# Eight convolution steps written out, with a third slot for the routed rows

## What is computed

```
w = softmax(weight, -1)                      # 8 heads x 7 taps
x = einsum('hk,bskhg->bshg', w, windows(x))  # causal, per head
for layer in (moe, moe2):
    logits = x @ w_gate
    e = argmax(logits); gate = softmax(logits)[e]
    x = gate * (relu(x @ w1[e]) @ w2[e])     # layer 2: also * sigmoid(x @ w_output_gate)[e]
```

## Time and profile before

| | |
|---|---|
| median of 3 timed runs | 1504.32 us (1502.03 to 1505.77) |
| profiled execution | 1496.17 us, span 1494.7 us, mean granted clock 0.916 |
| PE busy | 1249.3 us (84%) |
| DVE, ACT, POOL busy | 877.8, 635.4, 461.5 us |
| HBM over the span | 114 GB/s |

### The profile page before, as it was taken

How to read it: one execution, slowest core, us unless ns; L and a number is a source line. 1 busy time by engine, 2 the same in 40 slices (tenths; PEclk the granted TensorE clock), 3 DMA queues, 4 the chain that set the end, 5 groups by cost and what they waited for, 6 DMA issues and landing times.

```text
span 1494.7 us, 38165 instructions
## 1 busy us (share of the span) xinstructions
PE 1249.3 (84%) x13162; PEld 1155.2 (77%) x13162; DVE 877.8 (59%) x2364; ACT 635.4 (43%) x1126; POOL 461.5 (31%) x485
## 2 busy tenths in 40 slices
PE   0565664249999989999999999399999999999998
PEld 0554653249888878889888888299999999999997
DVE  4577777617888878887666666533333333333333
ACT  0456655314554544555444444133333333333333
POOL 3056756721333213332222222122222222222222
PEclk9867666579999999999999999599999999999999
DMA  4455765573757464746241411425244143313520
GB/s 135 133 178 186 231 203 185 179 211 84 188 146 218 119 188 134 225 123 191 42 133 43 141 38 33 158 52 140 49 141 142 46 143 84 106 48 99 176 62 21
DMA packets 202062, 192.55 MB, mean 129 GB/s; under 512 B 146142, under 2 KB 178554, under 8 KB 195872
## 3 DMA queue, kind: packets, MB, share of 16 engines
q1 hardware_dynamic: 176352, 127.72, 31.2%
q0 software_dynamic: 24512, 62.66, 13.2%
q10 hardware_dynamic: 1152, 1.59, 0.3%
HBM read 100.93 MB, written 68.96 MB: 114 GB/s over the span
## 4 chain that ended last, share of the span: by engine, by line
PE 56%; DVE 13%; issue 12%; ACT 5%; DMA 5%; POOL 4%; another core or an unknown queue 3%; SPq 1%; DVEq 0%; POOLq 0%; ACTq 0%
PE bank L665 55%; POOL rows L471 3%; DMA stage<-in_moe_w 2%; DVE am L889 2%; DVE hl L1072 2%; ACT rT L524 1%; ACT hh L605 1%; DVE xs L893 1%; DMA xT<-rows 1%; DMA rows<-rowa,idxa 1%; PE bank L670 1%; DVE band L877 1%; DVE split L973 1%; ACT conv L524 1%
## 5 line engine op out<-in xcount | busy, mean ns | idle before, releaser
L665 PE MATMUL bank<-xT,wslot 128*128 128x256 f16 x5040 | 607.0, 275 | 59.9 <-DMA xT<-rows 53.9
L1072 DVE SCALAR_TENSOR_TENSOR hl<-bank,hh 128x512 f16<-128x512 f32 x504 | 344.1, 690 | 410.8 <-ACT hh L605 383.5
L665 PEld LDWEIGHTS bank<-xT,wslot 128*128 128x128 f16 x5040 | 488.7, 98 | 118.9 <-DMA xT<-rows 54.3
L665 PE MATMUL bank<-wslot,hh 128*128 128x192 f16 x4032 | 525.8, 247 | 10.4 <-DVE hl L1072 4.5
L665 PE MATMUL bank<-wslot,hl 128*128 128x192 f16 x2016 | 497.6, 247 | 0.0
L605 ACT ACTIVATE hh<-bank 128x512 f16<-128x512 f32 x504 | 298.2, 598 | 388.4 <-PE bank L665 381.5
L665 PEld LDWEIGHTS bank<-wslot,hh 128*128 128x128 f16 x4032 | 363.0, 98 | 21.6 <-DVE hl L1072 8.4
L512 POOL DMA_INDIRECT out_tokens<-y,idxt x126 | 122.5, 972 | 415.8 <-ACT y L616 393.8
L485 POOL DMA_INDIRECT rows<-rowt,idxp x126 | 139.3, 1105 | 278.3 <-DVE idxp L950 247.6
L665 PEld LDWEIGHTS bank<-wslot,hl 128*128 128x128 f16 x2016 | 197.8, 98 | 0.1
L616 ACT ACTIVATE y<-bank,tf 128x192 f32<-128x192 f32 x252 | 92.1, 416 | 246.9 <-PE bank L665 210.0
(11 more groups left out here) (135 smaller groups left out, 843.4 us busy)
## 6 DMA issues: line engine op xcount, KB each, us to landing
wslot<-image SPq DMA_DIRECT2D x32, 1024.0 KB, 5.4
wslot<-image SPq DMA_DIRECT2D x32, 768.0 KB, 7.4
image<-split SPq DMA_DIRECT2D x8, 1024.0 KB
image<-split POOLq DMA_DIRECT2D x8, 1024.0 KB
xw<-in_x SPq DMA_DIRECT2D x4, 1536.0 KB, 13.2
stage<-in_moe_w SPq DMA_DIRECT2D x8, 768.0 KB
image<-split SPq DMA_DIRECT2D x8, 768.0 KB
stage<-in_moe_w POOLq DMA_DIRECT2D x8, 768.0 KB, 9.0
```

The lines of the kernel that those rows point to most:

```text
L665: return nc.tensor.matmul(o, a, b_, start=start, stop=stop, skip_group_check=True)
L1072: V.scalar_tensor_tensor(hl[:, c, :], bank[c][:, :], 0.0, hh[:, c, :], ALU.max, ALU.subtract).then_inc(hl_out, 1)
```

## The change

`steps` is a plain Python loop, so that all eight steps are straight code on every engine; the arithmetic that tied DVE's link semaphore to a loop counter goes. `rowa` and `idxa` get SLOTS = 3 slots, used as n % 3, with two scatter semaphores each; ACT's wait before its copies of step n is for the scatter of n-3 where it was n-2. For space, `xs` lies in slot 0 of `wslot` and the third `rowa` slot in slot 1 of it; the expert phase gets a small buffer `xsl` for its own scaled rows; and SP waits for the last step's `lo_ready` before the first load into `wslot`.

```diff
+SLOTS = 3
-        xs = sb("xs", [P, G, D], f32)
-        rowa = sb("rowa", [P, 2, G, RW], f32)
+        xsl = sb("xsl", [P, W2T, D], f32)
+        rowab = sb("rowab", [P, 2, G, RW], f32)
-        idxa = sb("idxa", [P, 2, G], i32)
+        idxa = sb("idxa", [P, SLOTS, G], i32)
         wslot = sb("wslot", [P, 2, WCOL], f16)
+        xs = wslot[:, 0, :].bitcast(f32)[:, 0:G * D].rearrange("p (w d) -> p w d", d=D)
+        rowa = [rowab[:, 0, :, :], rowab[:, 1, :, :],
+                wslot[:, 1, :].bitcast(f32)[:, 0:G * RW].rearrange("p (w c) -> p w c", c=RW)]
-        scat_a = [sem(f"scat_a{i}") for i in range(4)]
+        scat_a = [sem(f"scat_a{i}") for i in range(2 * SLOTS)]
         def steps(eng, body):
-            for q in range(SPB):
-                body(q, 0, q)
-            with eng.Fori(1, B) as b:
-                for q in range(SPB):
-                    body(b * SPB + q, b, q)
+            for n in range(STEPS):
+                body(n, n // SPB, n % SPB)
...
                     sp.wait_ge(dump_stored, 32)
+                    sp.wait_ge(lo_ready, STEPS)
...
                 for w in range(G):
                     nc.gpsimd.indirect_dma_start(
-                        rows[0][:, :], bass.IndirectOffsetOnAxis(idxa[0:WIN, q, w:w + 1], 0),
-                        rowa[0:WIN, q, w, :], None, bounds_check=ROWS - 1, oob_is_err=False).then_inc(scat_a[2 * q + w // (G // 2)], 16)
+                        rows[0][:, :], bass.IndirectOffsetOnAxis(idxa[0:WIN, n % SLOTS, w:w + 1], 0),
+                        rowa[n % SLOTS][0:WIN, w, :], None, bounds_check=ROWS - 1,
+                        oob_is_err=False).then_inc(scat_a[2 * (n % SLOTS) + w // (G // 2)], 16)
...
-            for i in range(4):
-                pool.wait_ge(scat_a[i], 8 * G * B)
+            for i in range(2 * SLOTS):
+                pool.wait_ge(scat_a[i], 8 * G * len(range(i // 2, STEPS, SLOTS)))
...
                 for half in range(2):
-                    if late(n, 2):
-                        act.wait_ge(scat_a[2 * q + half], b * 8 * G)
+                    if late(n, SLOTS):
+                        act.wait_ge(scat_a[2 * (n % SLOTS) + half], n // SLOTS * 8 * G)
                     ws = slice(half * G // 2, (half + 1) * G // 2)
-                    last = copy(rowa[0:WIN, q, ws, :].bitcast(f16)[:, :, 0:D], xs[0:WIN, ws, :])
+                    last = copy(rowa[n % SLOTS][0:WIN, ws, :].bitcast(f16)[:, :, 0:D], xs[0:WIN, ws, :])
...
-            dve_steps(n_here[0])
+            steps(dve, step)
```

More of the change, by code:

```diff
@@ L60 @@
 PER_QUAD = ((38, 40), (0, 0))
-PER_BATCH = 34
 EXPMASK = 0x7F800000
@@ L458, in step @@
                 if late(n, 1):
-                    scatter_step(n - 1, 1 - q)
+                    scatter_step(n - 1)
                 weight_maxima(n, q)
@@ L465, in weight_maxima, with scatter_step @@
                 nc.gpsimd.partition_all_reduce(wmx[:, slot, :], wam[:, slot, :], P, RMAX).then_inc(wmax_all, 1)
-            def scatter_step(n, q):
+            def scatter_step(n):
                 pool.wait_ge(index_ready, n + 1)
@@ L623, in row_hi @@
                         act.wait_ge(scat_p[v], i * 16 * W2T)
-                    copy(rowt[:, v, 0:n, :].bitcast(f16)[:, :, 0:D], xs[:, 0:n, :]).then_inc(hi_ready, 1)
+                    copy(rowt[:, v, 0:n, :].bitcast(f16)[:, :, 0:D], xsl[:, 0:n, :]).then_inc(hi_ready, 1)
                 def row_T(p, r):
@@ L706, in step, with step_logits @@
                 if late(n, 1):
-                    step_logits(n - 1, 1 - q)
-            def step_logits(n, q):
+                    step_logits(n - 1)
+            def step_logits(n):
                 def round_logits(r):
@@ L724, in step_logits @@
                     for i in range(RT):
-                        last = transposes(lambda c: dst[:, c, i, :], rowa[0:WIN, q, r * RT + i, :].bitcast(f16))
+                        last = transposes(lambda c: dst[:, c, i, :], rowa[n % SLOTS][0:WIN, r * RT + i, :].bitcast(f16))
                     last.then_inc(rT_done, 1)
@@ L738, in _ @@
             step_ranks(STEPS - 2)
-            step_logits(STEPS - 1, 1)
+            step_logits(STEPS - 1)
             step_ranks(STEPS - 1)
@@ L892, in scale_rows, with low_rows @@
             def scale_rows(nrows, nwins, src):
-                return V.scalar_tensor_tensor(xs[0:nrows, 0:nwins, :], src, CX,
+                return V.scalar_tensor_tensor(xsl[0:nrows, 0:nwins, :], src, CX,
                                               inv[0:nrows, 0:nwins].unsqueeze(2).broadcast_to((nrows, nwins, D)), ALU.mult, ALU.mult)
-            def low_rows(nrows, nwins, row):
-                V.tensor_tensor(row[:, :, D:D + DB], xs[0:nrows, 0:nwins, P:D], row[:, :, P:D], ALU.subtract)
-                return V.tensor_tensor(row[:, :, D + DB:2 * D], xs[0:nrows, 0:nwins, 0:P], row[:, :, 0:P], ALU.subtract)
+            def low_rows(scaled, row):
+                V.tensor_tensor(row[:, :, D:D + DB], scaled[:, :, P:D], row[:, :, P:D], ALU.subtract)
+                return V.tensor_tensor(row[:, :, D + DB:2 * D], scaled[:, :, 0:P], row[:, :, 0:P], ALU.subtract)
             def choose(nrows, nwins, bank_logits, gated):
@@ L985, in step_place @@
             def step_place(n, q):
-                factor(WIN, G, q, False, n + 2, rowa[0:WIN, q, :, MF:MF + 1])
+                factor(WIN, G, q, False, n + 2, rowa[n % SLOTS][0:WIN, :, MF:MF + 1])
                 dve.wait_ge(rank_done, n + 1)
-                place(WIN, G, rank_bank(G, RA), None, idxa[0:WIN, q, :]).then_inc(index_ready, 1)
+                place(WIN, G, rank_bank(G, RA), None, idxa[0:WIN, n % SLOTS, :]).then_inc(index_ready, 1)
             def step(n, b, q):
@@ L1007, in step @@
                 dve.wait_ge(hi_ready, n + 1)
-                row32 = rowa[0:WIN, q, :, :]
+                row32 = rowa[n % SLOTS][0:WIN, :, :]
                 V.tensor_copy(row32[:, :, MI:MI + 1], ids[0:WIN, :].unsqueeze(2))
-                low_rows(WIN, G, row32.bitcast(f16)).then_inc(lo_ready, 1)
+                low_rows(xs[0:WIN, :, :], row32.bitcast(f16)).then_inc(lo_ready, 1)
                 weights_max(q, None, None, 1)
@@ L1103, in low_out @@
                     V.tensor_copy(rowt[:, v, 0:n, MI:MI + 1], tidp[:, 0:n].unsqueeze(2))
-                    low_rows(P, n, rowt[:, v, 0:n, :].bitcast(f16)).then_inc(lo_ready, 1)
+                    low_rows(xsl[:, 0:n, :], rowt[:, v, 0:n, :].bitcast(f16)).then_inc(lo_ready, 1)
                 def choose_out(p):
```

2 lines of the change are left out of this document (1 added, 1 removed).

## The result

The changed kernel took 1495.26 us, the median of four runs (1491.05 to 1497.29), the kernel before 1505.05 (1502.03 to 1507.06) beside it: a ratio of 0.9933, 95% interval 0.9905 to 0.9961. That is 9.8 us less, where 1492.8 was predicted.

A forecast was written before the change was run, and what follows sets the result against it. Waits bound the convolution phase, TensorE the expert phase. Gains of 2.19 (step 2) and 9.34 (steps 3 to 5), together 11.5 us, took 1496.17 to 1484.7 profiled and the median 1504.32 to 1492.8 us; range 1481 to 1503.

The forecast's parts named there:

- (a): Steps 2, 4, 6, 7: ScalarE waits before row copies for the scatter of two steps ago; 20.7 us, predicted gone.
- the two us in step 2: Step 2 was to take 28.88 us, 2.19 less, because VectorE still gets its ranks at 109.36.
- (c): VectorE's wait for the logits in step 3, 6.04 us, and the like in step 5; predicted to go.
- (b): VectorE's wait for the ranks: 5.60 us in step 2, 4.20 in step 6, 2.61 in step 7.
- 15.88 us behind the burst: Rule that TensorE results still owed about 6 us into SyncE's burst of transfers arrive near 15.9 us into it.
- period of 27.47: Step 6's length, predicted for steps 3, 4 and 5 too: 91.75 us becomes 82.41, 9.34 less.
- The loop: Writing out the steps was costed at nothing, 0 to 1 us for all back edges; code fetches also at nothing.
- back-edge rival: The logits' wait is code awaited behind TensorE's loop branch; straight code removes it, 16 us less: 1488, chance 0.05.
- The end: GpSimd's end moves with step 7's start: step 7 at 232.4, scatter 7 about 273, expert phase from 305.7, lasting 1177.
- slower case: Code fetches queue behind full DMA engines, delaying release in five steps: 1508 at 3 us each, up to 1524; chance 0.10.
- Release sooner: TensorE's results are tied to ScalarE's stall, not the burst: 25.4 us a step, gain 23, 1481 us; chance 0.16.
- Replaced one for one: Logits in steps 3 and 5 still fall into the burst, ranks behind as now: 1498 to 1502 us, chance 0.21.

The follow-up runs named there:

- early weights: The changed kernel with the first expert's first weight load issued before the pad stores in the first layer: 1497.30 us, ratio 0.9920.
- ranks first: The changed kernel with TensorE doing the ranks ahead of both convolution halves, not between them: 1491.43 us, ratio 0.9871.
- held stores: Against the changed kernel: stage loads first, image stores and window load only after VectorE used the ranks; 1457.98 us (0.9904), on another chip 1495.83 us (0.9939).
- fifth chip: Chip of the fifth comparison, where the kernel with held stores ran again: 1495.83 us, ratio 0.9939; the kernel before took 1506.11 us.
- second profile: The changed kernel run and profiled again, unchanged, on the chip of the second comparison: 1495.36 us, ratio 0.9892.
- no weight loads: The changed kernel without the stage loads of the last five experts' weights in the first layer: 1492.60 us, ratio 0.9904.
- no window loads: The changed kernel without the loads of the input windows from step 4 on: 1490.62 us, ratio 0.9893.
- fourth chip: Chip of the fourth comparison, which ran kernels with stage loads first, held stores and no burst; the kernel before took 1471.61 us there.
- low rows first: The changed kernel with VectorE making the low parts of the rows before its wait for the ranks: 1511.97 us, ratio 1.0032.
- two-slot kernel: The changed kernel, steps still written out, with two slots for rows and indices instead of three: 1506.99 us, ratio 0.9987.

## Why the prediction was right, and where it wasn't

**The four waits (a), and the two us in step 2: right.** They are gone, and step 2 takes 28.74 us where 28.88 was worked out. That figure was in part luck: with early weights, ranks first and held stores (fifth chip) it was 28.88, 28.76 and 28.92, but in the changed kernel's second profile 31.82 and without weight or window loads 29.65 and 30.83. There the logits were held as in wait (c), which the prediction didn't expect in step 2.

**(b) takes the place of (c) at 15.88 us behind the burst: right in number, wrong in reason.** The period of 27.47 came out as 27.24 to 27.28 four times. As a clock the rule held from step 4 on in five other kernels or profiles on two more chips (second profile, early weights, ranks first, no weight loads, no window loads). But the prediction set the full DMA engines beside it, and full engines are neither needed through the wait nor enough for it: the distance holds with a DMA share of 0.35 (no weight loads), and with stores and window load moved away (held stores, fifth chip), and nothing is late at a share of 1.02 (fourth chip). Nor is the burst's start the clock: with the low rows first the ranks came 18.7 us behind it. In the kernels where the rule held, burst and scatters both follow the ranks of the step before at fixed distances, so either can serve as the clock; where they part, the results go with the scatters. That the 27.47 came out is right arithmetic on a distance whose reason was not known.

**The sum.** 11.5 us were predicted for the steps. It was 12.5 between the first profiles and 10.2 between the second ones (141.36 for 151.60 us), 11.6 between two and three slots by medians, and 9.8 and 13.4 between the medians of before and changed on the first and the second chip.

**The loop: right.** Nothing, by the two-slot kernel. More code packets are moved (29 on the first instruction queue for the 25 of the earlier trace rows), with no stall to see in the steps. The back-edge rival has fallen: the wait (c) is there in straight code too (6.78 us in step 3 with two slots). The rule of the Trainium skill (Runtime: NRT & Kernel Launch, Instruction fetch mechanics) on a taken branch, named with that rival, is not refuted by it; no row here shows such a stall.

**The end: right on average, missed in the profile.** The maximum of step 7 came at 234.11 for 232.4, as steps 0 and 1 ended 2.7 us later than in the earlier trace rows (the kernel before, profiled again, was 2.0 later too). Scatter 7 began at 273.93 for 273. The start at 305.7 and the 1177 us behind it rested on the profile of one short execution: it had 73.3 us from the maximum of step 7 to the first matmul, where the changed kernel took 77.8 and 75.4 and the kernel before, profiled again, 77.9. The changed kernel began the expert phase at 311.91 and 311.77. By the text's own mark, "longer by over 2 us", this looked like the slower case; the second profile of before shows that it is mostly not the change. Some 2 to 4 us stay open in the profiles; the medians, 9.8 to 13.4 us less, are too far apart to tell.

**The other rivals.** "Release sooner" (1481) didn't come: from step 3 on the ranks kept their distance to the burst. On the fourth chip, where nothing is held, two three-slot kernels had steps of 23 to 24.5 us, less than the 25.4 that this rival worked out, but the kernel before was faster there too and the ratio was 0.990 again (the changed kernel itself wasn't run on it). "Replaced one for one" needed logits late in steps 3 and 5; they weren't.

**What stays open** is why results of TensorE are held. Shown: it is no matter of its order, of weight or window loads, or of when stores are issued, and one kernel (held stores) has it on one chip and not on another. Not shown: the cause. No run took the whole burst out on a chip that holds results back, only its parts one at a time, and none touched the scatters. The traces also differ in the semaphore updates that they record. Of the 2048 that tell of the scatters' landings (16 for each of 128), the trace of held stores has 2011 on the fourth chip and 773 on the fifth; in the 10 us before each late delivery in steps 3 to 7 the traces of the changed kernel record 31 to 38 updates of any kind, the three on the fourth chip 141 to 212 before the ranks. Whether updates were held and merged there, or only their records lost, isn't shown, but it is where to look next: TensorE's results may be late because all such updates are. The one chip without the wait ran the kernel before 33 to 37 us faster. The Trainium skill (Perfetto Trace Analysis, Tensor Engine Instruction) says that a matmul's end in a profile is worked out from its size, while its semaphore is pushed only when PSUM has acknowledged the writes; that would allow results to be late behind records that look done, and no row here shows PSUM.

## What to carry to other kernels

Taking away a wait is worth what the next thing owed is late by: here 20.7 us of waiting gave some 12, and it could be worked out ahead from distances that repeat between rows. Such a distance is a number, not a cause: first measure it from everything else that has the same rhythm (here GpSimd's scatters fitted better than the burst that was tested), then test the cause with the suspect taken out, with the suspect present where the effect is absent, and on more than one chip. And profile the kernel before twice before a stage's length becomes a forecast.

## What the runs showed of the hardware

Chips differ. On those of the first, second, third and fifth comparison (1505 to 1509 us for the kernel before) the ranks' semaphore moved mostly 4.3 to 5.7 us after the recorded end of their matmuls, at most 7.8; on the fourth (1472 us) no semaphore of TensorE's in the convolution phase moved over 0.3 us late, and with the same source (held stores) the expert phase took 1172.2 us there and 1181.6 on the fifth, with the granted clock at 0.916 and 0.911 over the whole run. Where results came over 2 us late, their semaphores moved mostly 15.6 to 16.1, 17.2 to 17.5 or 18.6 to 18.8 us after VectorE had written the first low part of the weights, in kernels of different content; about one in five stood elsewhere, at 8.7 to 15.0 or 16.3. Nothing here explains that.
